# Attention blocks in pairs inside a fused attention, MLP and mixing kernel

## What is computed

```python
def _attn_ref(q, k, v, n_global, n_local):          # B, H, S, D = 2, 8, 768, 64
    scores = scale * np.matmul(q, k.transpose(0, 1, 3, 2))
    ...                                             # keep = first 8 keys, or 0 <= i - j < 96
    scores = np.where(keep, scores + bias, -1e9)    # bias = -slope of the head * distance
    a = np.exp(scores - np.max(scores, axis=-1, keepdims=True))
    a = a / (np.sum(a, axis=-1, keepdims=True) + 1e-09)
    return np.matmul(a, v)

def _moe_ref(x, g_ln, w_ch1, w_ch2):                # x: 2 x 768 x 512, w_ch1: 512 x 2048
    xn = (x - mu) / np.sqrt(var + 1e-06) * g_ln
    return x + np.maximum(xn @ w_ch1, 0.0) @ w_ch2

def _moe2_ref(x, w_theta, w_tok_r, w_tok_i, w_ch):
    theta = x @ w_theta
    u = x + w_tok_r @ (x * cos(theta)) + w_tok_i @ (x * sin(theta))
    return u + np.maximum(u @ w_ch, 0.0)
```

## Time and profile before

| what | value |
|---|---|
| time, median of 3 runs | 547.93 us (547.93 to 548.02) |
| the profiled execution, its own time | 548.37 us |
| its span in the profile | 546.6 us |
| PE busy | 536.8 us (98%) |
| DVE, ACT, POOL busy | 266.8, 173.0, 185.6 us |
| data read and written in HBM | 33.23 MB, 3.15 MB |

### The profile page before, as it was taken

One profiled execution on the slowest core, in us unless ns is written; L12 is line 12 of the kernel. 1 busy time (PEld: TensorE's weight loads), 2 busy tenths in 40 slices (PEclk: granted clock), 3 DMA queues, 4 the chain that ended last, 5 costly groups with the idle time before them and its releaser, 6 DMA issues.

```text
span 546.6 us, 8690 instructions
## 1 busy us (share of the span) xinstructions
PE 536.8 (98%) x3376; PEld 482.2 (88%) x3376; DVE 266.8 (49%) x678; ACT 173.0 (32%) x438; POOL 185.6 (34%) x165
## 2 busy tenths in 40 slices
PE   8899999999999999999999999999999999999997
PEld 7787888788888888999889998888799999999997
DVE  7665745646547454222221322355866669306054
ACT  5464444343535432110111111256555422001010
POOL 6596000000000000498000510033499798372500
PEclk9999999999999999999999999999999999999999
DMA  7663234132212000043100210000022133341202
GB/s 218 208 218 93 83 113 138 49 89 65 69 45 64 1 1 2 0 147 91 72 1 0 54 34 1 0 1 1 1 58 64 55 86 88 116 115 62 83 22 95
DMA packets 24810, 36.95 MB, mean 68 GB/s; under 512 B 2240, under 2 KB 17600, under 8 KB 24768
## 3 DMA queue, kind: packets, MB, share of 16 engines
q1 hardware_dynamic: 24768, 36.38, 21.6%
HBM read 33.23 MB, written 3.15 MB: 67 GB/s over the span
## 4 chain that ended last, share of the span: by engine, by line
PE 77%; issue 9%; POOL 9%; DVE 4%; ACT 0%; DVEq 0%; POOLq 0%; ACTq 0%
PE bank L1473 12%; PE bank L1089 12%; PE bank L1107 11%; PE bank L882 11%; PE bank L865 10%; PE bank L1491 6%; POOL trig L1234 4%; PE bank L505 4%; PE bank L535 4%; POOL ring_l L1217 3%; PE bank L520 3%; PE bank L1325 3%; POOL ring_h L1214 2%; PE bank L893 1%; PE bank L545 1%
## 5 line engine op out<-in xcount | busy, mean ns | idle before, releaser
L865 PE MATMUL bank<-xnT,w1h 128*128 128x256 f32 x384 | 73.3, 290 | 1.3 <-DVE xnT L826 1.3
L1089 PE MATMUL bank<-xnT,w1h 128*128 128x384 f32 x256 | 65.2, 335 | 0.0
L1473 PE MATMUL bank<-ring_h,z_hi 128*128 128x384 f32 x192 | 64.8, 338 | 0.2 <-POOL ring_l L1217 0.2
L1473 PE MATMUL bank<-ring_h,z_lo 128*128 128x384 f32 x192 | 64.2, 334 | 0.0
L1473 PE MATMUL bank<-ring_l,z_hi 128*128 128x384 f32 x192 | 64.1, 334 | 0.0
L865 PEld LDWEIGHTS bank<-xnT,w1h 128*128 128x128 f32 x384 | 59.4, 191 | 5.3 <-issue 3.7
L795 POOL TENSOR_TENSOR rstd<-rtmp,minus_half 128x2 f32<-128x2 f32 x6 | 4.2, 699 | 154.1 <-DVE rtmp L766 154.1
L1234 POOL TENSOR_TENSOR trig<-x,trig 128x512 f32<-128x512 f32 x24 | 32.8, 1390 | 67.6 <-ACT trig L1281 67.6
L484 ACT ACTIVATE sp_buf<-sp_buf,row_max 128x256 f32<-128x256 f32 (+1 forms) x96 | 46.1, 483 | 29.8 <-DVE row_max L428 29.8
L865 PE MATMUL bank<-xnT,w1l 128*128 128x256 f32 x192 | 54.2, 282 | 0.0
L1217 POOL TENSOR_TENSOR ring_l<-raw,ring_h 128x768 fp32r<-128x768 f32 x24 | 48.0, 1998 | 2.0
(11 more groups left out here) (124 smaller groups left out, 1124.3 us busy)
## 6 DMA issues: line engine op xcount, KB each, us to landing
raw<-wtokT SPq DMA_DIRECT2D x24, 384.0 KB, 3.2
raw<-w SPq DMA_DIRECT2D x8, 1024.0 KB, 5.5
v_sb<-vwin SPq DMA_DIRECT2D x16, 256.0 KB, 2.7
k_sb<-kcols SPq DMA_DIRECT2D x16, 200.0 KB, 3.2
q_sb<-qT SPq DMA_DIRECT2D x24, 128.0 KB, 2.8
outT<-out_sb SPq DMA_DIRECT2D x16, 192.0 KB, 1.8
v_sb<-vwin SPq DMA_DIRECT2D x8, 192.0 KB, 3.3
k_sb<-kcols SPq DMA_DIRECT2D x8, 136.0 KB, 3.1
```

What stands on the lines that cost most here:

```text
L865: last = nc.tensor.matmul(bank_of(n)[:, 0:AN], wt[q][:, d, f * P:(f + 1) * P], xnT[:, AT * c:AT * c + AT, low, d, :], start=(d == 0 and m ...
L1089: last = nc.tensor.matmul(h_bank[f % 2][:, 0:CN], wt[slot][:, d, fs], tokens(low, d), start=first, stop=(d == DC - 1 and wt is w1l))
L1473: last = nc.tensor.matmul(bank, zt[b][:, s, r, ds], wt[j % RING][:, r, :], start=(s == 0 and r == 0 and m == 0), stop=(s == TILES - 1 and ...
```

## The change

Inside the loop the blocks go in pairs (4 and 5, 6 and 7, and so on). At one step PE runs the second products of blocks k and k+1 and right behind them the scores of blocks k+2 and k+3.

- Both results of a pair stand in bank 4, side by side, are copied out at once (`copy_attnT_pair`, 512 columns), transposed back into the same bank over themselves (`transpose_back_pair`) and written with one instruction (`write_x_pair`).
- Scores of even blocks go to banks 0 and 1, of odd blocks to banks 2 and 3, and the transposed probabilities go into the same banks as the block's scores.
- The `output` group 10 of each third (`BESIDE`) and the fourth of the first transposes take bank 4 instead of their turn in banks 5 to 7; each user of a bank now waits for the last user of that bank.
- The scores of block 5 move ahead of the loop, beside those of block 4, and its loads move forward.
- On POOL the root of the second third moves ahead of the last half of the split of `raw` 3.
- The statistics of a third stand two steps earlier (three in the first third).

```diff
+            if k < PAIRS:
+                return banks[5:7] if k in (1, 3) else banks[0:2]
+            return banks[0:2] if k % 2 == 0 else banks[2:4]
+        def pT_banks(k):
+            return banks[2:4] if k < PAIRS else score_banks(k)
...
-        SCORES_AT = {place_at(k, (-12, -4, 0, 8)): k for k in range(8, BLOCKS)}
...
-        ATTEND_AT.update({5: 4, 8: 5, 11: 6, 15: 7})
...
+        ATTEND_AT = {5: 4, 12: 6, **{place_at(k, (0, 0, 10, 0)): k for k in range(8, BLOCKS, 2)}}
+        SCORES_AT = {s: k + 2 for s, k in ATTEND_AT.items() if k + 2 < BLOCKS}
+        BACK_AT = {s + 1: k for s, k in ATTEND_AT.items()}
+        TRANSPOSE_AT = {2: 4, 4: 5, 9: 6, 11: 7, **{place_at(k, (-6, -3, 4, 7)): k for k in range(8, BLOCKS)}}
+        MASKS_AT = {s + n: k + n for s, k in SCORES_AT.items() for n in range(2)}
+        EXPS_AT = {s + 3 * n: k + n for s, k in SCORES_AT.items() for n in range(2)}
+        SECOND_EXPS_AT = {s + 2: k for s, k in EXPS_AT.items()}
+        SECOND_MASKS_AT[1], EXPS_AT[1], SECOND_EXPS_AT[2] = 5, 5, 5
...
             load_qk(4)
+            load_qk(5)
...
+        def copy_attnT_pair(act, k):
+            act.wait_ge(attnT_ready, k + 2)
+            nc.scalar.activation(attnT[:, :], banks[4][:, :], ACT.Copy).then_inc(attnT_copied, 2)
...
+        def transpose_back_pair(pe, k):
+            pe.wait_ge(attnT_copied, k + 2)
+            for j in range(2 * AT):
+                last = nc.tensor.transpose(banks[4][:, j * P:(j + 1) * P], attnT[:, j * P:(j + 1) * P], ident[:, :])
...
+                if k >= 2 * PAIRS and k % PAIRS == 0:
+                    pe.wait_ge(turn_out, turn["group", k // PAIRS - 2, BESIDE] + 1)
...
+            alone = n == DC - 1 or (kind == "group" and m == BESIDE)
+            bank = banks[4] if alone else turn_bank[(n - turn_banks.count(banks[4])) % 3]
...
-            split_raw(pool, 3)
+            split_raw(pool, 3, (0, 1))
+            norm_root(pool, 1)
+            split_raw(pool, 3, (2, 3))
...
+                if n == turn["group", c, BESIDE] and c + 1 < EARLY:
+                    pe.wait_ge(x_written, PAIRS * (c + 2))
...
             scores(pe, 4)
+            scores(pe, 5)
...
                 if s in ATTEND_AT:
                     attend(pe, ATTEND_AT[s])
+                    attend(pe, ATTEND_AT[s] + 1)
...
                 if s in SCORES_AT:
                     scores(pe, SCORES_AT[s])
+                    scores(pe, SCORES_AT[s] + 1)
```

More of the change, by code:

```diff
@@ L345, in early_sync @@
             load_v(4)
[L346 to L349, removed]
+            raws = {7: 2, 8: 3, 12: 4, 14: 5}
+            for k in range(6, BLOCKS + 1):
+                if k < BLOCKS:
+                    load_qk(k)
+                load_v(k - 1)
                 if k in raws:
@@ L491, in copy_attnT, with write_x_pair @@
                 act.wait_ge(attn_ready, k)
-            nc.scalar.activation(attnT[:, :], o_bank(k)[:, 0:AN], ACT.Copy).then_inc(attnT_copied, 1)
+            nc.scalar.activation(attnT[:, 0:AN], o_bank(k)[:, 0:AN], ACT.Copy).then_inc(attnT_copied, 1)
+        def copy_attnT_pair(act, k):
[5 more added lines that the diff above has]
+                last = nc.tensor.transpose(banks[4][:, j * P:(j + 1) * P], attnT[:, j * P:(j + 1) * P], ident[:, :])
+            last.then_inc(attn_ready, 2)
+        def write_x_pair(dve, k, other):
+            r = AT * (k % DENS)
+            dve.wait_ge(den_step, 2 * k + 4)
+            dve.wait_ge(attn_ready, k + 2)
+            to = other * (BATCH * UNITS - AT * k) + AT * k
+            nc.vector.tensor_tensor(
+                x[:, bass.ds(to, 2 * AT), :].rearrange("p u (h d) -> p (u h) d", h=2),
+                banks[4][:, :].rearrange("p (h d) -> p h d", d=DH),
+                inv[:, r:r + 2 * AT, :].rearrange("p u h -> p (u h)").unsqueeze(2).broadcast_to([P, 4 * AT, DH]),
+                ALU.mult).then_inc(x_written, 2)
         def scores(pe, k):
             t, s = place(k)[1], k % SLOTS
-            if k >= 2:
-                pe.wait_ge(masked_ready, 2 * AT * (k if k > PAIRS else k - 1))
+            if k > PAIRS:
+                for u in range(AT):
+                    pe.wait_ge(probsT_copied[u], k - 1)
+            elif k >= 2:
+                pe.wait_ge(masked_ready, 2 * AT * (k - 1))
             pe.wait_ge(q_loaded[s], 16 * (k // SLOTS + 1))
@@ L708, in output_group, with wait_for_bank @@
             return turn["group", c, q * (FC + AT) + FC + i]
+        BESIDE = EARLY_QUARTERS * (FC + AT) - AT
+        turn_banks, free_at = [], []
+        for n, (kind, c, m) in enumerate(turn):
+            alone = n == DC - 1 or (kind == "group" and m == BESIDE)
+            bank = banks[4] if alone else turn_bank[(n - turn_banks.count(banks[4])) % 3]
+            users = [i for i, b in enumerate(turn_banks) if b is bank]
+            free_at.append(0 if alone or not users else users[-1] + 1)
+            turn_banks.append(bank)
         def bank_of(n):
-            return banks[2] if n == DC - 1 else turn_bank[n % 3]
+            return turn_banks[n]
+        def wait_for_bank(pe, n):
+            if free_at[n]:
+                pe.wait_ge(turn_out, free_at[n])
         def mlp_sync(sp):
@@ L732, in early_pool @@
             split_raw(pool, 2)
-            split_raw(pool, 3)
-            for c in range(1, EARLY):
+            split_raw(pool, 3, (0, 1))
+            norm_root(pool, 1)
+            split_raw(pool, 3, (2, 3))
+            for c in range(2, EARLY):
                 norm_root(pool, c)
@@ L1039, in early_vector @@
                     invert_den(dve, TRANSPOSE_AT[s])
-                if s in SCORES_AT:
-                    masks(dve, SCORES_AT[s], (0,))
         def h_low(dve, done, fs=range(FC)):
```

67 lines of the change are left out of this document (33 added, 34 removed).

## The result

| | before | after |
|---|---|---|
| time, median, same chip | 547.97 us (547.93 to 548.02) | 538.95 us (538.89 to 539.12) |
| profiled execution, own time | 548.37 us | 538.95 us |
| its span | 546.6 us | 537.1 us |
| PE busy | 536.8 us | 529.4 us |
| first hidden product of the loop | 27.94 us | 27.37 us |

The ratio is 0.9836, interval 0.9819 to 0.9853. Forecast were 538.9 us; the total came out as said, and the way to it only partly.

A forecast was written before the change was run, and what follows sets the result against it. PE's own queue was taken as the bound (busy 98%, full clock). 548.37 - 6.7 - 2.95 - 0.5 + 1.0 + 0.1 = 539.3 us profiled, less 0.44 to the median: 538.9 us, range 537.0 to 542.2.

The forecast's parts named there:

- What one costs, how many visits: PE in the loop: 62 changes of form become 29; 33 go at 0.203 us each, 6.7 us gained.
- the first rival: The 0.2 us belong to each block's product, not the change of form: 2.5 us gained, 543.1 us; chance 0.09.
- The wait at the end of a third: Group 11's wait for DVE's addition to x goes in five thirds, 0.59 us each, 2.95 us gained.
- New waits at the start: Steps 2 and 4: PE waits for exponentials of blocks 4 and 5, 1.0 us lost, bounds 0 to 1.5.
- Before the loop: Block 5's scores, moved ahead, fill PE's 0.41 us wait for normalized rows; gain 0.4 to 0.65, taken 0.5 us.
- ACT's burst: ACT gets two blocks at once; at a third's start its exponentials still come in time, with cover 0.4 us.
- late exponentials: Rival: second transposes of each of nine pairs wait 0.3 us for ACT, 2.7 us lost, 541.6 us; chance 0.14.
- the chain: Rival: ACT's late exponentials hold hidden read-outs and then PE, 1.5 us for each of nine visits, 552.4 us; chance 0.04.
- the 0.1 for all new waits in the loop: DVE and ACT get two blocks in a burst; 0.1 us lost in all, later read-outs harmless.
- POOL: Root ahead of the last two parts of raw 3's split: PE's third part has cover 2 us, so nothing lost.
- The sum: 548.37 - 6.7 - 2.95 - 0.5 + 1.0 + 0.1 = 539.3 us profiled, 538.9 us as median.

The follow-up runs named there:

- e1: Changed kernel with each pair's second products and scores alternating on PE in nine visits, 18 more changes of form: 542.75 us.
- e2: Changed kernel with the second block of each pair moved one step later on PE, 29 more changes of form: 545.14 us.
- e8: e3 with POOL's old order, that is e4 without bank 4 for group 10: 545.86 us.
- e9: e8 with the transposes of probabilities of blocks 9, 13, 17 and 21 at step 20 of a third in place of 21: 542.62 us.
- e7: e4 with the pieces of blocks 4 to 7 one or two steps later: 537.07 us.
- e6: Changed kernel with the scores of block 5 back in the loop, alone, ahead of step 1: 538.88 us.
- e5: Kernel before with only POOL's part of the change, the second third's root ahead of the last half of raw 3's split: 549.16 us.
- e4: Changed kernel with POOL's old order, the whole split of raw 3 and then the second third's root: 538.24 us.
- e3: Changed kernel with group 10 of each third back in the turn of banks 5 to 7, without bank 4's two waits: 549.56 us.

## Why the prediction was right, and where it was not

**What one costs, how many visits: held.** Forecast were 33 changes of form at 0.203; e1 measured 0.205, and e2, with its two other differences taken out, 0.203. So 6.8 for 6.7. A merged visit was to take 4.4 us, 4.8 by the first rival; it takes 4.42.

**The wait at the end of a third: held, and too narrow.** 0.59 each came back whole when the bank was taken away (0.94 or 0.95 for 0.35 in each of the five thirds of e8 and e9), so 2.95 stands. What failed is the step that priced only this. In the kernel before, group 10 also wrote the bank of group 9. Four times the visit at step 20 covered that; the count of visits has this visit among those that go, and did not ask what it had covered. The fifth time, at 206.95, nothing covered it and 0.73 us was lost that the forecast should have claimed. Without bank 4 the change gives 545.86 us with POOL in its old order, 542.62 with e9's cover as well, and with POOL's part no gain at all (549.56).

**New waits at the start: held in size.** 1.13 for 1.0. In part it came from a reason that I had not worked out. The first tile's transposes, not only the second's, waited, and the wait named is `row_max` of DVE: the transposes now overwrite the block's own scores, so they need both tiles' masks done. e7 shows the term as a whole.

**Before the loop: held, as one half of a trade; a gain beside it was missed.** PE's wait of 0.41 us for the normalized rows was filled: e6 starts the loop 0.23 earlier, where the step's own numbers say 0.21 to 0.46 (0.86 less 0.65 or 0.4). But the scores taken out of the loop had stood where the next wait arises, and e6 puts the net within 0.1 us of nothing. The step treated a piece's place as free once the piece was gone. The missed gain is in the other wait, 1.29 us before and 0.94 in all kernels with pairs. In the kernel before, the fourth of the first transposes had bank 2, not a turn in banks 5 to 7, and was counted in the turn all the same, so the first hidden group took the bank of the second transposes and waited for two of DVE's read-outs. Now the fourth is not counted, the group takes the bank of the first and waits for one. The transposes start at 25.10 in e5 and at 25.09 in e6, the loop at 27.50 and 27.14: 0.36 us. This is read from the kernels and the rows; no experiment undoes it alone.

**ACT's burst: held. DVE's: too small.** There is no wait at L552 after 60 us, so the rivals of late exponentials and of the chain have no place (the chain's work adds up to 6.3 us and not 6.7, which makes it no likelier). But the 0.1 for all new waits in the loop was 0.45. The step said of the late read-outs only that a hidden bank is wanted three groups on. Group 5 is `output`, its read-out is DVE's, and three groups on, group 8 came 0.1, 0.1 and 0.25 late behind it (161.60 above). e2, where the statistics come behind the read-out, has no such place.

**POOL: failed.** "Cover 2 us, so nothing" looked at one consumer, PE's third part of `raw` 3, and no product waits for `w2l`, as said. The cost came by another way, DVE: 0.7 us by e4, 0.81 in its loop.

**The sum.** In the loop: 6.8 for the form, 0.86 for block 5's products, 2.95 and 0.73 for the bank, less 1.13, 0.81 and 0.45, makes 8.95; measured is 208.95 - 200.06 = 8.89. Ahead of it 0.36 are gained and 0.23 paid, 0.13. Together 9.02, and the medians are 547.97 - 538.95 = 9.02 apart. So nearly nothing is left over, but the forecast did not know these terms. It was too low by 0.73 for bank 4, 0.36 and 0.13 before the loop and 0.1 for the form, 1.3 in all, and too high by 0.81 for POOL, 0.35 for DVE's burst and 0.13 for the new waits, 1.3 again. That is luck, and the nearness of 538.95 to 538.9 is no evidence for the steps. The loop's start, 0.57 earlier after, is not a clean reading: it lies between 27.4 and 27.9 in kernels whose work ahead of the loop is the same (27.37 after, 27.86 in e1; 27.94 before, 27.50 in e5). The scores of the first two blocks, at about 4.8 us, take 2.27 us in after and 2.72 before, which is about the 0.4 by which the profiled execution of before was over its median; in e1, e2 and e5 the list names waits of 0.2 to 0.8 for loads of keys between 6 and 8 us. Why the loads land apart I did not test.

## What to carry to other kernels

Where one engine is the bound, read the distance between starts and price its borders, then group equal pieces. For each piece that is moved or merged away, ask what it had covered at its old place, for a bank as much as for a queue: here one bank, with POOL's move beside it, decided between 1.6% and nothing. And work that is moved on an engine with slack must be held against what runs beside it at the new time, not only against its own consumer.

## What the runs showed of the hardware

- A change between 128 x 128, 128 x 64 and 64 x 128 costs PE 0.20 us each way (0.205 over 18 in e1, 0.203 over 29 in e2). Blocks of one form in a row cost nothing between them.
- Some of DVE's work on SBUF is slow beside POOL's subtractions: two scalings of 128 x 512 took 2.02 us together in after instead of 0.99 in e4, a step on two columns 1.16 instead of 0.16, and e3 and e5 show the same (1.99 and 1.97 for the scalings, 1.16 and 1.13 for the step). POOL's subtractions hardly changed, 1.26 to 1.34 us beside it and 1.27 alone. DVE's read-outs of a bank (L895, L897, and L847 in e5) stayed at 0.39 to 0.42 us in the same stretch. The Trainium skill ("SBUF — State Buffer", Who interferes with whom) calls the port pair that the two engines share an exclusive lock, which a DVE instruction needs when it has two inputs in SBUF or runs in a 2-port mode. The trace agrees: in after the step that starts at 57.53 ends with POOL's instruction, at 58.7, and in e5 the one from 62.14 ends at 63.27, POOL's at 63.24.
- After 3.4 us without a product (e3), the granted clock was 0.60 over the stretch from 64 to 68 us, with 0.50, the 1.2 GHz level, from 64 to 67, and it was 1.00 again from 68. An idle time of 1.2 us (e8) had no such effect: the clock was 1.00 in all its stretches from 56 to 72 us. But a stretch with only short waits can lose it too: in e5's profiled execution it was 0.50 from 28 to 30 us, behind waits of 0.41 and 1.29, and the kernel before had the same two waits and 1.00. What makes the difference stays open.
- A wait in the list counts from a modelled end: it has 0.35 for a loss of 0.59, and 0.50 for 0.74. The distances between starts give the loss.
